# Order and slots of the Strassen weight preparation in a fused attention and two-layer feed-forward kernel

## What is computed

```python
# attention in chunks of 32 queries; keys: 8 memory keys + 16 to the left + the chunk + 8 to the right
scores = scale * np.matmul(q_c, k_full.transpose(0, 1, 3, 2))
a = np.exp(scores - max) ; a = a / (sum + 1e-09)
out[:, :, c_start:c_end] = np.matmul(a, v_full)
x = attention output as (3072, 512)
h = x @ w_in;   g = where(h > 0, h, exp(min(h, 0)) - 1);   x = g @ w_out        # layer 0
h = x @ w_in2;  g = s * max(h, 0)**2 + b;                  return g @ w_out2    # layer 1
```

## Time and profile before

| | |
|---|---|
| time, median of 3 runs | 1150.56 us (1150.12 to 1152.0) |
| the profiled execution's own time | 1150.04 us |
| its span, first to last instruction | 1148.1 us |
| mean granted TensorE clock | 0.991 |
| busy: TensorE (matmul), VectorE, ScalarE, GpSimd | 1098.3, 849.4, 772.6, 391.6 us |
| instructions | 18176 |
| bytes read from and written to device memory | 226.10 and 75.50 MB |

### The profile page before, as it was taken

How to read it: one execution, slowest core, us unless ns; L and a number is a source line. 1 busy time by engine, 2 the same in 40 slices (tenths; PEclk the granted TensorE clock), 3 DMA queues, 4 the chain that set the end, 5 groups by cost and what they waited for, 6 DMA issues and landing times.

```text
span 1148.1 us, 18176 instructions
## 1 busy us (share of the span) xinstructions
PE 1098.3 (96%) x5787; PEld 875.2 (76%) x5787; DVE 849.4 (74%) x1258; ACT 772.6 (67%) x1818; POOL 391.6 (34%) x427
## 2 busy tenths in 40 slices
PE   7899888989999999989999999999999999999998
PEld 4677666767777777778788787887888888888886
DVE  5696686468887956898878968968848579576475
ACT  4797786677657757757758667666666467674564
POOL 5679789741331432236275113653000000000000
PEclk9899999999999999999999999999999999999999
DMA  9998999999789889869899789898697666776664
GB/s 209 258 269 256 339 336 351 346 291 327 229 252 253 256 248 271 274 209 334 304 356 343 238 262 369 300 355 272 187 283 227 191 195 189 219 216 193 193 190 158
DMA packets 204054, 302.80 MB, mean 264 GB/s; under 512 B 112824, under 2 KB 121016, under 8 KB 203960
## 3 DMA queue, kind: packets, MB, share of 16 engines
q1 hardware_dynamic: 203960, 301.65, 85.4%
HBM read 226.10 MB, written 75.50 MB: 263 GB/s over the span
## 4 chain that ended last, share of the span: by engine, by line
PE 72%; ACT 7%; DVE 6%; DMA 5%; issue 5%; POOL 3%; SPq 3%; ACTq 0%; POOLq 0%; DVEq 0%
PE ps L1002 35%; PE ps L987 30%; DMA w_scratch<-w_new 3%; ACT ps L1082 2%; PE ps L902 2%; DMA w_ring<-w_scratch 1%; DVE g_lo L1463 1%; POOL w_new L789 1%; PE ps L927 1%; ACT elu L1168 1%; PE ps L954 1%; PE ps L896 1%; POOL att L789 1%; ACT elu L1173 1%; PE ps L911 1%
## 5 line engine op out<-in xcount | busy, mean ns | idle before, releaser
L987 PE MATMUL ps<-xc_hi,w_ring 128*128 128x512 f32 x1344 | 434.7, 396 | 6.0 <-DVE X L1432 2.8
L1002 PE MATMUL ps<-g_hi,w_ring 128*128 128x512 f32 x1344 | 421.2, 395 | 14.3 <-issue 9.1
L1002 PEld LDWEIGHTS ps<-g_hi,w_ring 128*128 128x128 f32 x1344 | 249.6, 189 | 73.0 <-issue 14.2
L987 PEld LDWEIGHTS ps<-xc_hi,w_ring 128*128 128x128 f32 x1344 | 253.2, 188 | 64.0 <-issue 2.9
L1002 PE MATMUL ps<-g_lo,w_ring 128*128 128x512 f32 x672 | 263.2, 392 | 0.0
L987 PE MATMUL ps<-xc_lo,w_ring 128*128 128x512 f32 x672 | 262.5, 391 | 0.0
L789 POOL TENSOR_TENSOR w_new<-w_raw,w_new 128x256 fp32r<-128x256 f32 x179 | 167.2, 940 | 218.6 <-ACT w_new L1221 215.4
L1463 DVE TENSOR_TENSOR g_lo<-X,g_hi 128x512 fp32r<-128x512 f32 x240 | 176.9, 742 | 24.4 <-ACT g_hi L1207 23.7
L1207 ACT ACTIVATE g_hi<-X 128x512 fp32r<-128x512 f32 x240 | 149.0, 628 | 57.2 <-PE ps L1002 54.6
L1380 DVE TENSOR_TENSOR X<-s,ps 128x512 f32<-128x512 f32 x144 | 96.2, 682 | 104.3 <-ACT s L1144 78.0
L1002 PEld LDWEIGHTS ps<-g_lo,w_ring 128*128 128x128 f32 x672 | 126.7, 189 | 26.9
(11 more groups left out here) (124 smaller groups left out, 1337.8 us busy)
## 6 DMA issues: line engine op xcount, KB each, us to landing
w_ring<-w_scratch SPq DMA_DIRECT2D x336, 512.0 KB, 4.5
w_scratch<-w_new SPq DMA_DIRECT2D x179, 256.0 KB, 5.2
w_scratch<-att SPq DMA_DIRECT2D x45, 256.0 KB, 5.2
w_raw<-in_moe_w_in SPq DMA_DIRECT2D x16, 512.0 KB, 5.7
w_raw<-in_moe_w_out SPq DMA_DIRECT2D x16, 512.0 KB, 5.8
x_scratch<-y SPq DMA_DIRECT2D x12, 512.0 KB, 6.3
att<-x_scratch SPq DMA_DIRECT2D x12, 512.0 KB, 6.7
out<-elu SPq DMA_DIRECT2D x24, 256.0 KB, 4.4
```

What stands on the lines that cost most here:

```text
L987: last = nc.tensor.matmul(bank_of(st.pi, st.i), w[:, a, cols], x[:, st.pi, kk, :], start=(st.pi in (P1, P5, P4) and kk == 0 and n == 0), s ...
L1002: last = nc.tensor.matmul(bank_of(st.pi, d), w[:, a, cols], x[:, k % RING, :], start=(st.pi in (P1, P5) + (P4,) * (1 - st.gr) and st.i == ...
```

## The change

The order of the products in a set becomes P1, P4, P2, P7, P5, P6, P3. In GpSimd's program the second, third and fourth sums follow P2's low half; P7, P5, P6 and P3 follow the sums. The slots of ScalarE's cuts, which stood 0.9 steps apart, come in the pattern 0, 0.6, 1.2, 1.8, 4.3, 4.9, 5.5 with 6.3 steps from set to set, and for the pair of sets 14 and 15 in a list of its own. The slots of layer 1 (`pp >= PRODUCTS`) stay.

```diff
--- before.py
+++ after.py
@@ -54,7 +54,9 @@
           (P4, 0, 10), (P4, 1, 11), (P4, 2, 14), (P4, 3, 15))
 SUMS = [(pi, j) for pi, j, _ in SUM_AT]
 RAW_OF = {P1: X11, P3: X22, P2: X21, P6: X22, P7: X12, P5: X11, P4: X21}
-PREPARED = (P1, P4, P7, P2, P5, P6, P3)
+PREPARED = (P1, P4, P2, P7, P5, P6, P3)
+CUT_AT = (0, 0.6, 1.2, 1.8, 4.3, 4.9, 5.5)
+CUT_PAIR_AT = (0, 0.6, 3, 3.6, 4.2, 4.8, 5.4, 6, 9, 9.6, 10.2, 10.8, 11.4, 12)
 RING = 4
 W_RING = 4
 SAVES = 4
@@ -198,8 +200,11 @@
 
 def hi_slot(pp):
 
+    if pp < 7 * PAIR:
+        k, o = divmod(pp - HEAD_PREP, 7)
+        return int(7 + 6.3 * k + CUT_AT[o])
     if pp < PRODUCTS:
-        return 7 + (pp - HEAD_PREP) * 9 // 10 + (3 if pp >= PREP_AT[PAIR + 1, P1] else 0)
+        return int(7 + 6.3 * (PAIR - HEAD_PREP // 7) + CUT_PAIR_AT[pp - 7 * PAIR])
     if pp < WIDE_END:
         return PER_TILE + 4 + (pp - PRODUCTS) * 3
     t, j = divmod(pp - WIDE_END, 42)
@@ -795,19 +800,19 @@
                     nc.gpsimd.tensor_tensor(a21, a11, a21, ALU.subtract).then_inc(w_sums, 1)
                     for pi in (P1, P4):
                         split_w(m, pi)
+                for m in ms:
+                    split_w(m, P2)
                 for m, (a11, a12, a21, a22) in zip(ms, blocks):
                     pool.wait_ge(w_sums, sums_count(m, 1))
                     nc.gpsimd.tensor_tensor(a22, a22, a21, ALU.subtract).then_inc(w_sums, 1)
                 for m, (a11, a12, a21, a22) in zip(ms, blocks):
                     pool.wait_ge(w_sums, sums_count(m, 2))
                     nc.gpsimd.tensor_tensor(a11, a22, a11, ALU.add).then_inc(w_sums, 1)
-                for pi in (P7, P2, P5, P6):
+                for m, (a11, a12, a21, a22) in zip(ms, blocks):
+                    nc.gpsimd.tensor_tensor(a12, a12, a22, ALU.subtract).then_inc(w_sums, 1)
+                for pi in (P7, P5, P6, P3):
                     for m in ms:
                         split_w(m, pi)
-                for m, (a11, a12, a21, a22) in zip(ms, blocks):
-                    nc.gpsimd.tensor_tensor(a12, a12, a22, ALU.subtract).then_inc(w_sums, 1)
-                for m in ms:
-                    split_w(m, P3)
 
             def sums_of_x(t):
                 n = HEAD_SUMS + 8 * (t - 1)
```

## The result

The changed kernel took 1159.74 us (median of 8 runs, 1156.29 to 1164.04), the kernel before 1151.76 us beside it (8 runs, 1148.28 to 1154.04): ratio 1.0079, 95% interval [1.0057, 1.0101]. The forecast was no change, 1150.5 us, with a range up to 1154.2. The profiled execution took 1160.3 us; its span is 1158.5 us against 1148.1, so 10.4 us are to be found in it.

A forecast was written before the change was run, and what follows sets the result against it. Bound: TensorE's early waits on ScalarE, held by GpSimd's sums, with the DMA queue full. Terms +5.3 - 4.4 - 0.9 = 0.0 us against 1150.04 profiled, so 1150.5 us by median; own range 1148.3 to 1152.7, all cases 1145.2 to 1154.2.

The forecast's parts named there:

- What bounds the kernel: Up to about step 70: TensorE waits for ScalarE, held by GpSimd's sums, full DMA queue and set 15's raw load.
- The sums move ahead: Sets prepared up to step 66: cuts find their sums done, and ScalarE loses 23.7 us of waiting.
- a sign of being wrong: ScalarE at P5's cut: waits for sums reappearing there would show the forecast wrong.
- could win the 11.4 us: TensorE ahead of step 62: 8.0 us of waits and 3.4 us from the lower clock could be had.
- Who takes over: DMA, 113.6 to 242 us: at 352 GB/s instead of 340, set 15's load lands 4.4 us earlier.
- the lower bound: Landing of set 15's load: only the queue's dip at 149.9 to 151.4 us is filled, 0.9 us earlier.
- the waits only change their names: Rival, ahead of step 62: ScalarE's cuts wait for buffers instead of sums, TensorE's gaps stay; 1154.0 us, chance 0.06.
- Buffers: every product keeps 6.3 steps: Weight buffers: each product stays 6.3 steps behind the one before it in its buffer, so no cost.
- Set 15's cuts: Slots 66 to 70: cuts ahead of their data put 8.5 us before the attention output, was 3.2; costs 5.3 us.
- Afterwards: Slots 70 to 82: doubled fourth sum holds no cut, four cuts fewer, lesser TensorE waits go; gains 0.9 us.
- What costs nothing: Bursts of cuts, SyncE standing at P7's save, buffers, layer 1's swap and the head's sets: priced at no cost.
- The chance for slower: Slower by over 0.2%: 0.28, from set 15's load deciding (0.22) and waits only changing names (0.06).

The follow-up runs named there:

- the second execution: The changed kernel once more, unaltered, profiled beside the kernels of a later chip session: 1.0064 of the kernel before.
- the kernel with the later saves: Changed kernel with SyncE's saves of the pair's two P7 put behind the ring load of steps 78 and 79: 1.0039 of the kernel before.
- the later comparison: Changed kernel run again unaltered (1.0064) against it with the saves of the pair's two P7 behind the ring load of steps 78 and 79 (1.0039).

## Why the prediction was wrong, step by step

**What bounds the kernel: right.** ScalarE's sum waits, the queue at over 1 of its time, and the raw load of set 15 were the three things at work.

**"The sums move ahead": right for ScalarE, and worth nothing.** All 23.7 us of sum waits went in the profiled execution; 2.3 us until the third sum came back in the second, and 7.8 in the kernel with the later saves, at the very cut, P5's, that the prediction had named as a sign of being wrong. That TensorE "could win the 11.4 us" did not follow: its waits from 137 to 226 us stayed (8.0, then 9.0 us), and so did its stretches at the lower clock ahead of step 62 (one of 6.8 us for two of 3.4).

**"Who takes over", -4.4 us: this is the first step that failed.** It reasoned that a queue fed more closely would reach 352 GB/s over the whole stretch. It moved 343, and the load of set 15 landed 0.4 us later, not 4.4 earlier. The six executions with the new order and slots moved 336 to 345 GB/s, the three with the old 339 to 346. Measured against step 12, the six have it land after 119.3 us in the mean, the three after 118.7. Even the lower bound, 0.9 earlier, was too high. The 352 GB/s were a reading of 26 us, taken for that of 128: in the changed kernel the same 26 us moved 367 GB/s, with TensorE busy for only 21.33 of them, and the whole stretch no more. What happened instead is what the prediction gave a chance of 0.06, "the waits only change their names": the waits for saves rose from 7.2 to 22.4 us. Its evidence stood in the earlier trace rows, at the very line whose sum waits were taken away. "Buffers: every product keeps 6.3 steps" put this at nothing; it counts the steps between two uses of a buffer and not when the save in between lands.

**Set 15's cuts, +5.3 us: right in mechanism, a little large.** The 8.5 us between cut and attention output were 8.47 in both executions, and ScalarE's wait was 8.0 (7 or more foretold). TensorE stood 5.9 and 7.6 us around step 70 (some 8 foretold). It lost 4.0 and 4.6 us from step 66 to 72, since in the kernel before part of that path was not waited for. By the ratios the slots cost 0.0047 with half the ring's traffic, and 0.0025 between the kernels with the pair's sums behind P7, where the intervals overlap.

**"Afterwards", -0.9 us: not there.** The lesser waits, 0.4 us at step 81 and 0.5 at step 82, are the same in the changed kernel. Steps 72 to 90 without the late ring load took 32.1 us against 32.4. (The two differences as printed make 1.0, not 0.9.)

**"What costs nothing": the second step that failed.** The prediction saw that "SyncE can stand at that save with the next ring load behind it" and let "the ring's lead of three pairs of steps" cover it. It reckoned with a microsecond or two, for the three sums of a single set. In the pair there are six sums, 6.5 us, ahead of P7's low half, and they fall behind a start that set 15's wait had already delayed; the ring load came 3.75 us after its slot was free, and the attention loads behind it took the rest of the lead. This cost 2.7 us of waiting and half of 6.8 us at the lower clock in the first execution, and 2.5 to 3 us in the later comparison. The bound given for it ("the landing gains only the lower bound") looked at the wrong place, ahead of step 70 and not behind it. What it says of layer 1, "P7 and P2 swap, beside an unbroken TensorE", failed too: the stand at P7's save is there as well, with a wait of 1.3 to 1.8 us at step 362, and the kernels with the new order lose some 1.8 us behind step 90.

**The sum.** Put with what was measured: +0.3 up to step 66, +4.0, +5.7 and +0.4 make the 10.4 us of the profiled execution, where the prediction had -4.4, +5.3 and -0.9. One term was not there at all (-4.4 measured as +0.3 up to step 66), and one that was there, the late ring load, was missing. The chance for slower, 0.28, was on the right side, but its cases ended at 1154.2 because they all shared the zero for SyncE. That the waits for saves and the late ring load would add up was in none of them.

## What to carry to other kernels

A wait that is removed is worth what the next limit leaves of it: where the same instruction already waits for something else now and then, that is the next limit. An instruction placed ahead of its data on an in-order engine costs the wait and all that stands between it and the next consumer; placing it and the cuts after it behind that consumer was worth 0.3% here. When work moves ahead on one engine, look at which in-order queue waits for what it was moved ahead of, and price it for the largest case (here a pair of sets), together with the delays that the same change brings there.

## What was not expected of the hardware

- Behind a wait of 2.67 us at step 84 TensorE ran 6.8 us at the granted clock 0.50 (1.2 GHz) though it was busy all the time. In the second execution of the same kernel the 2.6 us wait at that place was followed by no such stretch, and its loss from step 72 to 90 was smaller (2.5 against 5.7 us).
- SyncE's issue of the same small attention load, the memory keys beside steps 75 to 77, took 2.33 us in the changed kernel, 1.40 in the kernel before, and 0.65 in the kernel before with half the ring's traffic. It varies as much within one execution (0.5 to 2.6 us in the kernel before). This delays everything that follows in its program.
- With half the ring's bytes the kernel before was faster by only 0.8%, though its DMA share in the stretch fell from 1.05 to 0.91: taking load off the queue ended the wait for set 15 (66 to 72 in 12.4 us) and won 2.9 us behind step 90, while steps 12 to 66, where ScalarE still waited for sums, gained only 0.8 us.
